# Attention in front of two expert layers: q in 1 KB runs, score groups over two row tiles, denominators from a tiny column

## The chip, the cores and the metric

The kernel runs on one core of a Trainium2 chip. The metric is the device time of one execution in microseconds (us). Of the kernel before there are three runs, 450.9, 451.15 and 452.35 us, with a median of 451.15 us. One execution was taken by the hardware profiler; its times are those of the rows below.

Names of the engines: PE is the matrix engine (TensorE), PEld its weight loads, DVE the vector engine, ACT the scalar engine, POOL is GpSimd, SP the engine that issues most DMAs. A row of the profile names the line of the kernel (L1475 is line 1475), the operation, and the tiles that are written and read.

## The reference, cut to what matters

```python
def _attn_ref(q, k, v):            # (8, 8, 576, 64): batch, head, token, dim
    k_p = k.reshape(B, H, 72, 8, D).mean(axis=3)
    v_p = v.reshape(B, H, 72, 8, D).mean(axis=3)
    scores = scale * np.matmul(q, k_p.transpose(0, 1, 3, 2))
    attn = np.exp(scores - np.max(scores, axis=-1, keepdims=True))
    attn = attn / (np.sum(attn, axis=-1, keepdims=True) + 1e-09)
    return np.matmul(attn, v_p)

def _moe_ref(x, phi, w1, w2):      # x: (4608, 512), 8 experts of 4 slots
    logits = x @ phi
    d = softmax(logits, axis=0);  c = softmax(logits, axis=1)
    slot_input = (d.T @ x).reshape(8, 4, 512)
    slot_out[e] = np.maximum(slot_input[e] @ w1[e], 0.0) @ w2[e]
    return c @ slot_out.reshape(32, 512)

def _moe2_ref(x, w_in, w_out, g_ln):
    h = x @ w_in
    solu = h * softmax(h)
    return (layer_norm(solu) * g_ln) @ w_out
```

Keys and values are averaged over 8 tokens, so a row of scores has 72 entries for each head. The first layer's dispatch softmax `d` runs over all tokens of all batches.

## The kernel before, in words

All data is float32. Three stages follow each other.

**Attention, batch by batch (to some 178 us).** A batch has 576 tokens in five row tiles. Tiles 0 to 3 have 128 rows, row p of tile t being token 4p + t; tile 4 holds the last 64 tokens, four heads on partitions 0 to 63 and four on 64 to 127. q comes in four DMAs of 256 KB a batch (runs of 64 numbers, 256 B) and two of 64 KB for tile 4; each of the five has a semaphore of its own. k and v come as two DMAs each, are folded in three levels (`fold`: levels 0 and 1 of width 1280 and 640, level 2 of 320) by POOL, a few of them by DVE, and are transposed by PE (`kT_t`, `vT_t`). ACT copies kT into `kblk`: for each of four pairs of heads a block diagonal of 128 rows and 2 x 72 columns, so one matmul gives the scores of two heads. The softmax tile `attn` has for each row tile four pairs of 147 columns: one column of ones, and for each head 72 scores and one column that holds 1e-9 (`TINY`).

For each tile the steps are these, and each engine runs them in an order written out by hand (`step(b, par, t)` on every engine, t from 1 to 5, where t = 5 is tile 0 of the next batch):

- PE `qT_t` (L1393): transposes q, four pairs of heads; ACT `qT_evac` copies the result to SBUF
- PE `scores` (L1412, tile 4: L1408); DVE `sub_max` takes the maximum (L1033) and subtracts it while writing into `attn` (L1039); ACT `exps` (L728); DVE `sums` takes the sum (L1046) and the reciprocal (L1051)
- POOL `norm` (L577) multiplies `attn` with the reciprocals and counts `attn_ready` up by one
- PE `aT_t` (L1475, tile 4: L1471) waits for `attn_ready` and transposes the 588 columns of the tile in blocks of 128; ACT `aT_evac` copies them
- PE `lt_t` (L1499) gives the logits with the v-weighted phi (`vphi`), ACT `lt_evac`, PE `l_t` (L1506), DVE `logit_evac` (L1058)

In step t, PE issues in this order: qT(t+3), scores(t+2), lt(t-1), aT(t), l(t-1), with `kT_t`, `vT_t`, `wphi_t`, `vphi_t`, `v72_t`, and the dispatch work of the batch before (`dat_t`, `datT_t`, `slot_t`, `lmax_t`, `mb_t`) between them. In step t, POOL issues norm(t+1), and behind it the folds: `v_fold` levels 1 and 2 in step 1, `k_fold` level 0 in step 3, levels 1 and 2 in step 4, `v_fold` level 0 in step 5. DVE begins step t with sums(t+1) and sub_max(t+2); in step 1 `vphi_evac` stands before them and `new_max` (L1083, L1087) behind them, in step 4 of the batches from 1 on `vT_copy` (L1065) stands at the end. ACT copies one half of kT in step 1 and one in step 2, before `lt_evac` and `exps` of the step.

`dat_t` multiplies the dispatch weights with `attn`, whose column of ones gives the denominator of the dispatch softmax.

SP issues the loads in one queue: at the start k(0), q tiles 0 and 1, v(0), q tiles 2 and 3, then, as POOL and DVE free the buffers, k(1), the rest of q(0), q tile 0 of batch 1, v(1), the rest of q(1), k(2). From batch 3 on it also loads expert weights into free places; ten halves of 2 MB fit before PE has used the first. The start has instructions of its own: at its end PE issues scores(2), vT_t, aT(0) of batch 0, and then step 1. There are a few transposes without use (`keep_clock`, L1560) in its gaps.

**Expert layer (to some 222 us).** PE multiplies the slots with w1 and w2 of each expert (`hid_t` L1698, `so_t` L1720). The load of weight half n (L446, L436, L438) waits until PE has used the half n - 10.

**Output layer (to the end).** 36 tiles of 128 tokens; the products of L1835 to L1837 keep PE full.

Of the kernel before, what the change touches and what calls it, by code (L numbers as in the profile page):

```python
# [29 lines left out]
F32 = mybir.dt.float32  # L30
F32R = mybir.dt.float32r
ALU = mybir.AluOpType
# [3 lines left out]
P = 128  # L36
B, H, S, D = 8, 8, 576, 64
POOL = 8
# [14 lines left out]
PAIR = 1 + 2 * HEAD  # L53
# [28 lines left out]
def build(nc, q, k, v, phi, w1, w2, w_in, w_out, g_ln, out):  # L82
    with ExitStack() as ctx:
# [36 lines left out]
        qb, ql = [bump("qb0", [P, 4, DM])], [bump("ql0", [P, DM])]  # L120
# [9 lines left out]
        qb.append(bump("qb1", [P, 4, DM]))  # L130
# [4 lines left out]
        kblk = [bump("kblk0", [P, PAIRS, 2 * SP])]  # L135
# [7 lines left out]
        kblk.append(bump("kblk1", [P, PAIRS, 2 * SP]))  # L143
# [9 lines left out]
        alpha = [bump(f"alpha{i}", [P, 1]) for i in range(2)]  # L153
        dlog = bump("dlog", [P, TILES, SLOTS])
# [29 lines left out]
        col_parts = bump("col_parts", [P, DM])  # L184
        m_hi = bump("m_hi", [P, FF // 4], F32R)
# [9 lines left out]
        csum = bump("csum", [P, B * TILES])  # L195
        csum1 = bump("csum1", [P, B * TILES])
        crec = bump("crec", [P, B * TILES])
# [5 lines left out]
        hid = [bump(f"hid{i}", [P, 2 * P]) for i in range(2)]  # L203
        hz = [bump(f"hz{i}", [P, FC, SLOTS]) for i in range(2)]
        pick = bump("pick", [P, 4, 5 * SLOTS], F32R)
        c_first = bump("c_first", [P, 2 * P])
# [37 lines left out]
        q_main = q[:, :, 0:4 * P, :].rearrange("b h (p t) d -> b t p h d", t=4)  # L244
# [72 lines left out]
        def head_sums(par, t):  # L317

            return pair_rows(par, t)[:, :, 1:].rearrange("p j (h c) -> p j h c", c=HEAD)

        def head_cols(par, t):
            return head_sums(par, t)[:, :, :, 0:SP]
# [25 lines left out]

        def kblk_half(par, hh):
            return kblk[par][hh * D:(hh + 1) * D, :, hh * SP:(hh + 1) * SP]  # L350
# [49 lines left out]
        def _(sp):  # L400
# [23 lines left out]
            def load_q(b, par, tiles=range(TILES)):  # L424
                for t in tiles:
                    if t < 4:
                        sp.dma_start(qb[par][:, t, :].rearrange("p (h d) -> p h d", h=H), row(q_main[:, t], b)).then_inc(sem(f"q_in{par}{t}"), 16)
                        continue
                    for hh in range(2):
                        sp.dma_start(ql[par][LEFT * hh:LEFT * (hh + 1), 0:DM // 2].rearrange("p (h d) -> p h d", d=D),  # L430
                                     row(q_left[:, :, H // 2 * hh:H // 2 * (hh + 1), :], b)).then_inc(sem(f"q_in{par}{t}"), 16)
# [36 lines left out]
            for b in range(1, 7):  # L468
# [4 lines left out]
                if b >= 3:  # L473
                    load_w((b - 3) // 2, (b - 3) % 2)
# [1425 lines left out]
```

## Time and profile before

| what | value |
|---|---|
| median of three runs | 451.15 us (450.9 to 452.35) |
| span of the profiled execution | 449.2 us |
| busy in the span: PE, PEld | 431.4 us (96%), 335.0 us (75%) |
| busy: DVE, ACT, POOL | 316.9 (71%), 267.4 (60%), 251.0 us (56%) |
| chain that ended last | PE 75%, DVE 7%, ACT 6%, DMA 6%, issue 3% |
| DMA | 91.71 MB in 125951 packets, 105176 of them under 512 B |
| granted TensorE clock, mean | 1.000 |

Busy time is the time in which an engine has an instruction under way. The shares are means over the three stages; the text on a stage reads that stage. In a timeline row the first number is the start in us from the span's start and the second the duration; x5 means that five instructions in a row are merged, and what stands in brackets is the idle time just before on that engine and who ended it.

### The profile page before, as it was taken

Reading aid. Unit: us, or ns where it says so; the run is one execution under the profiler, and the core shown is the slowest. Engines: PE = TensorE matmul, PEld = TensorE weight load, DVE = VectorE, ACT = ScalarE, POOL = GpSimd, SP = SyncE. Lnnn points to the kernel's source line nnn. Section 1 sums busy time; section 2 is a strip of 40 time slices with the busy share of each in tenths; the row PEclk is TensorE's granted clock in tenths of the full one; section 3 lists DMA queues with packets and bytes.
Section 4 is the critical chain, followed back from the end, with each engine's and each line's share of the span. In section 5 each row is a group of like instructions: output and inputs, shape, how many; then the busy total and the mean of one; then the engine's idle time right before and its main releaser. Section 6 shows DMA issues by size and latency. Waiting matters only on the chain.

```text
span 449.2 us, 10103 instructions
## 1 busy us (share of the span) xinstructions
PE 431.4 (96%) x3492; PEld 335.0 (75%) x3492; DVE 316.9 (71%) x558; ACT 267.4 (60%) x604; POOL 251.0 (56%) x347
## 2 busy tenths in 40 slices
PE   6899999999999998999899999999999999999997
PEld 6676787778778775445578788888888888888886
DVE  5888697877879665736598987777777777777311
ACT  2588878778787854134387665655565555666310
POOL 2569977878887230112034336766766667666540
PEclk9999999999999999999999999999999999999999
DMA  8969959898999998999500276676666766666642
GB/s 258 296 190 239 257 151 267 329 283 279 341 211 359 388 393 285 392 389 396 207 1 24 48 163 118 132 144 137 134 136 140 141 134 134 132 118 136 154 81 47
DMA packets 125951, 91.71 MB, mean 204 GB/s; under 512 B 105176, under 2 KB 105440, under 8 KB 124000
## 3 DMA queue, kind: packets, MB, share of 16 engines
q1 hardware_dynamic: 120752, 82.08, 66.8%
q10 hardware_dynamic: 5168, 9.24, 6.0%
q8 instruction: 17, 0.28, 0.3%
q14 instruction: 14, 0.11, 0.1%
HBM read 66.13 MB, written 9.44 MB: 168 GB/s over the span
## 4 chain that ended last, share of the span: by engine, by line
PE 75%; DVE 7%; ACT 6%; DMA 6%; issue 3%; POOL 1%; SPq 1%; DVEq 0%; ACTq 0%
PE banks L1835 13%; PE banks L1837 13%; PE banks L1836 13%; PE banks L1412 5%; DMA wslot<-in_moe_w 5%; PE banks L1475 3%; PE banks L1393 3%; PE banks L1807 3%; ACT vpad L685 2%; PE banks L1499 2%; PE banks L1535 2%; PE banks L1698 2%; PE banks L1506 2%; PE banks L1720 2%; DVE attn L1039 1%
## 5 line engine op out<-in xcount | busy, mean ns | idle before, releaser
L1835 PE MATMUL banks<-wo_hi,uh 128*128 128x512 f32 x280 | 109.6, 391 | 0.1
L1837 PE MATMUL banks<-wo_hi,ul 128*128 128x512 f32 x280 | 109.0, 389 | 0.0
L1836 PE MATMUL banks<-wo_lo,uh 128*128 128x512 f32 x280 | 108.9, 389 | 0.0
L653 POOL TENSOR_TENSOR ul<-u_col,uh 128x1024 fp32r<-128x1024 f32 x30 | 72.2, 2407 | 16.2 <-ACT uh L685 15.0
L577 POOL TENSOR_TENSOR attn<-attn,srec 128x576 f32<-128x576 f32 (+1 forms) x40 | 43.2, 1082 | 39.6 <-DVE srec L1051 39.4
L950 ACT ACTIVATE sq<-u,st 128x1024 f32<-128x1024 f32 x36 | 41.5, 1153 | 39.9 <-DVE u L1284 39.9
L1835 PEld LDWEIGHTS banks<-wo_hi,uh 128*128 128x128 f32 x280 | 52.6, 188 | 11.4 <-DVE ul L1301 0.5
L1837 PEld LDWEIGHTS banks<-wo_hi,ul 128*128 128x128 f32 x280 | 52.5, 188 | 11.0
L1836 PEld LDWEIGHTS banks<-wo_lo,uh 128*128 128x128 f32 x280 | 52.6, 188 | 10.7
L1284 DVE SCALAR_TENSOR_TENSOR u<-banks,ex 128x1024 f32<-128x1024 f32 x35 | 42.7, 1223 | 22.3 <-ACT ex L941 22.2
L1274 DVE TENSOR_REDUCE st<-banks 128x1 f32<-128x1024 f32 x35 | 42.6, 1218 | 17.5 <-PE banks L1807 17.5
L941 ACT ACTIVATE ex<-banks,st 128x1024 f32<-128x1024 f32 x35 | 39.0, 1114 | 17.1 <-DVE st L1274 16.7
L685 ACT ACTIVATE uh<-u_col 128x1024 fp32r<-128x1024 f32 x30 | 31.8, 1060 | 28.4 <-DMA u_col<-u_blk 14.5
L1315 DVE TENSOR_SCALAR osb<-banks,rs 128x512 f32<-128x512 f32 x35 | 26.0, 742 | 19.2 <-PE banks L1837 19.2
L1412 PE MATMUL banks<-kblk,qT 128*128 128x144 f32 x256 | 37.8, 291 | 1.0 <-DVE attn L1039 0.9
L1294 DVE STREAM_TRANSPOSE u_blk<-u 128x1024 f32<-128x1024 f32 x30 | 37.4, 1246 | 1.9
L1412 PEld LDWEIGHTS banks<-kblk,qT 128*128 128x128 f32 x256 | 33.1, 190 | 3.7 <-issue 3.5
L639 POOL TENSOR_SCALAR st<-st 128x1 f32<-128x1 f32 x36 | 6.9, 190 | 51.6 <-ACT sq L950 51.3
L1033 DVE TENSOR_REDUCE smax<-banks 128x8 f32<-128x576 f32 (+1 forms) x40 | 27.4, 685 | 10.9 <-PE banks L1412 10.5
L728 ACT ACTIVATE attn<-attn 128x576 f32<-128x576 f32 (+1 forms) x40 | 25.5, 636 | 14.8 <-DVE attn L1039 14.4
L1046 DVE TENSOR_REDUCE ssum<-attn 128x8 f32<-128x584 f32 (+1 forms) x40 | 27.8, 694 | 4.9 <-ACT attn L728 4.6
L685 ACT ACTIVATE aT<-banks 128x512 f32<-128x512 f32 (+1 forms) x80 | 28.7, 403 | 2.1 <-PE banks L1475 1.0
(197 smaller groups left out, 792.8 us busy)
## 6 DMA issues: line engine op xcount, KB each, us to landing
wslot<-in_moe_w SPq DMA_DIRECT2D x13, 2048.0 KB, 13.6
u_col<-u_blk SPq DMA_DIRECT2D x240, 64.0 KB, 2.2
qb<-in_q SPq DMA_DIRECT2D x32, 256.0 KB, 6.3
out<-osb ACTq DMA_DIRECT2D x32, 256.0 KB, 2.5
vraw<-in_v SPq DMA_DIRECT2D x8, 640.0 KB, 5.4
kraw<-in_k SPq DMA_DIRECT2D x7, 640.0 KB, 5.9
vraw<-in_v SPq DMA_DIRECT2D x8, 512.0 KB, 4.0
kraw<-in_k SPq DMA_DIRECT2D x7, 512.0 KB, 5.0
```

Source lines behind the costliest of these rows:

```text
L577: pool.tensor_tensor(a, a, per_head(srec[bit(tile)], t)[:, :, :, None].to_broadcast([P, tile_pairs(t), 2, SP]), ALU.mult) \
L653: pool.tensor_tensor(ul[par][:, :, :].rearrange("p c (q t) -> p (c q) t", q=4), v, uh[par][:, :, :].bitcast(F32).rearrange("p c (q t) -> p ...
L685: return act.activation(o, i, ACT.Copy, scale=scale)
L941: act.activation(ex[par][:, :, :], h_banks(par), ACT.Exp, bias=st[k % STATS]["nmax"][:, :], accum_out=st[k % STATS]["den"][:, :]).then_inc ...
L950: act.activation(sq[par][:, :], u[k % URING][:, :], ACT.Square, scale=-float(FF), bias=st[k % STATS]["usum"][:, :], accum_out=st[k % STATS ...
L1274: dve.tensor_reduce(st[k % STATS]["nmax"][:, :], h_banks(k % 2), AX.XY, ALU.max, negate=True).then_inc(sem("nmax"), 1)
L1284: dve.scalar_tensor_tensor(u[k % URING][:, :].rearrange("p (a n) -> p a n", a=2), h_banks(par), 1.0, ex[par][:, :, :], ALU.mult, ALU.mult, ...
L1294: dve.transpose(u_blk[slot][:, :, :, k % 2, :].rearrange("p c q t -> p (c q) t"), u[k % URING][:, :].rearrange("p (b f) -> p b f", f=BLK)) \
L1412: last = pe.matmul(s_view[:, j, 0:2 * SP], qT[bit(tile)][:, j, :], kblk[par][:, j, :], start=True, stop=True)
L1835: pe.matmul(ps[4 + par], uh[par][:, c, :], wo_hi[:, c, :], start=(c == 0), stop=False)
L1836: pe.matmul(ps[4 + par], uh[par][:, c, :], wo_lo[:, c, :], start=False, stop=False)
L1837: last = pe.matmul(ps[4 + par], ul[par][:, c, :], wo_hi[:, c, :], start=False, stop=(c == FC - 1))
```

## The change

1. q of a batch comes in one DMA of 1 MB: partition p gets for each head the tokens 4p to 4p + 3, a run of 256 numbers (1 KB). For batch 0 it is cut in two DMAs of 512 KB (runs of 512 B), token offsets 0 and 1 first; tile 0 now waits for 512 KB. SP issues all of q(1) ahead of v(1).
2. A group of scores ("unit") takes four heads of two token offsets instead of eight heads of one. Unit t of the first four has heads 4(t mod 2) to 4(t mod 2) + 3 of the offsets 2(t div 2) and the next. The transposed q has on its 128 rows one head at two offsets, so `kblk` holds for each head a block diagonal of that head twice: 8 blocks in place of 4. ACT's and DVE's copies of kT have twice the elements (64x256 where they had 64x128). The tile of 64 rows takes its pairs out of the same buffer with a stride of three.
3. The unit writes into `attn` its half of the columns of two row tiles. `sub_max`, `exps`, `sums` and `norm` work on `unit_cols` or `unit_sums`, four heads x two tiles x 72 (73) columns. `aT_t` of row tile 0 waits for the norms of units 0 and 1, that of tile 1 too; tiles 2 and 3 wait for units 2 and 3 (`units_of`).
4. The column of ones goes. The denominators are the sums over a TINY column, divided by TINY at the end. A pair has 146 columns, the row tile 584, its last block 72 (from 76).
5. Three small buffers of the later stages lie elsewhere (`hid`, `c_first`, `csum` and its kin).

The order of instructions on PE, DVE, ACT and POOL is as before.

```diff
-        q_main = q[:, :, 0:4 * P, :].rearrange("b h (p t) d -> b t p h d", t=4)
+        q_main = q[:, :, 0:4 * P, :].rearrange("b h (p t) d -> b p h (t d)", t=4)
...
+        def unit_sums(par, t):
+            if t == TILES - 1:
+                return pair_rows(par, t).rearrange("p j (h c) -> p j h c", c=HEAD)
+            first = GROUP_HEADS * HEAD * (t % 2)
+            return attn[:, par, t - t % 2:t - t % 2 + 2, first:first + GROUP_HEADS * HEAD].rearrange("p a (h c) -> p h a c", c=HEAD)
+        def unit_cols(par, t):
+            return unit_sums(par, t)[:, :, :, 0:SP]
+        def units_of(b, t):
+            return b * TILES + (TILES if t == TILES - 1 else t - t % 2 + 2)
...
         def kblk_half(par, hh):
-            return kblk[par][hh * D:(hh + 1) * D, :, hh * SP:(hh + 1) * SP]
+            return kblk[par][hh * D:(hh + 1) * D, :, hh, :]
+        def kblk_pair(par, j):
+            return kblk[par][:, 2 * j:2 * j + 2, :, :].rearrange("p h a c -> p (h a) c")[:, 0::3, :]
...
+            def load_q(b, par):
+                sp.dma_start(qb[par][:, :, :], row(q_main, b)).then_inc(sem(f"q_in{par}"), 16)
+            def load_first_q(n):
+                c = slice(2 * D * n, 2 * D * (n + 1))
+                sp.dma_start(qb[0][:, :, c], row(q_main, 0)[:, :, c]).then_inc(sem("q_in0" if n else "q_first"), 16)
...
             load_first_k()
-            load_q(0, 0, (0, 1))
+            load_first_q(0)
             load_v(0)
-            load_q(0, 0, (2, 3))
+            load_first_q(1)
...
-            load_q(0, 0, (4,))
-            load_q(1, 1, (0,))
+            load_left_q(0, 0)
             sp.dma_start(g8[:, :], g_v).then_inc(sem("g_in"), 16)
             sp.wait_ge(sem("v_pooled"), 1)
+            load_q(1, 1)
             load_v(1)
-            load_q(1, 1, (1, 2, 3, 4))
+            load_left_q(1, 1)
...
-                a = head_cols(tile[1], t)
+                a = unit_cols(tile[1], t)
                 pool.wait_ge(sem("srec"), num(tile) + 1)
...
-                dve.memset(pair_cols[:, :, :, 0], 1.0)
...
-                    i = ql[par][:, j * P:(j + 1) * P] if t == 4 else qb[par][:, t, j * P:(j + 1) * P]
+                    i = ql[par][:, j * P:(j + 1) * P] if t == 4 else qb[par][:, GROUP_HEADS * (t % 2) + j, P * (t // 2):P * (t // 2 + 1)]
...
-                        last = pe.matmul(s_view[:, j, 0:2 * SP], qT[bit(tile)][:, j, :], kblk[par][:, j, :], start=True, stop=True)
+                        last = pe.matmul(s_view[:, j, 0:2 * SP], qT[bit(tile)][:, j, :],
+                                         kblk[par][:, GROUP_HEADS * (t % 2) + j, :, :].rearrange("p a c -> p (a c)"), start=True, stop=True)
...
             def aT_t(tile):
-                pe.wait_ge(sem("attn_ready"), num(tile) + 1)
+                pe.wait_ge(sem("attn_ready"), units_of(b, t))
```

## Rows read from the trace of the kernel before

**Rows 1.** The page's first part: busy us, share of the span, instructions.

```profile
PE 431.4 (96%) x3492; PEld 335.0 (75%) x3492; DVE 316.9 (71%) x558; ACT 267.4 (60%) x604; POOL 251.0 (56%) x347
```

**Rows 2.** The chain of work that ended last: start, duration, what.

```profile
195.80 20.35 DMA wslot<-in_moe_w
```

**Rows 3.** Timeline of SP: the first weight load that waits for PE's products.

```profile
179.31 1.77 SPq L446 DMA_DIRECT2D wslot<-in_moe_w  x4
```

**Rows 4.** Windows: busy by engine, then PEclk, DMA share, GB/s.

```profile
75.00:150.00 75.00, 73.53 (x909) 58.02 (x910) 60.97 (x140) 59.29 (x183) 57.05 (x41) 1.00 0.97 304
90.00:95.00 5.00, 4.87 (x63) 3.54 (x61) 2.98 (x7) 3.75 (x12) 4.11 (x4) 1.00 1.25 231
140.00:145.00 5.00, 5.00 (x60) 3.69 (x60) 4.83 (x12) 3.71 (x12) 4.74 (x5) 1.00 1.03 409
175.00:180.00 5.00, 4.71 (x83) 3.04 (x75) 3.31 (x11) 2.14 (x5) 0.00 (x0) 1.00 0.68 188
```

**Rows 5.** Timeline: scores of tile 1, its norm, and the transposes of tile 0.

```profile
72.07 1.25 PE L1412 MATMUL banks<-kblk,qT 128*128 128x144 f32 x8
...
77.10 1.15 POOL L577 TENSOR_TENSOR attn<-attn,srec 128x576 f32<-128x576 f32 x1 [1.60 <-DVE srec L1051]
...
77.44 0.77 PE L1475 MATMUL banks<-ident,attn 128*128 128x128 f32 x5
```

**Rows 6.** Timeline: the norm of tile 3 and the transposes of tile 2.

```profile
83.39 1.06 DVE L1087 TENSOR_TENSOR slot_max<-lmax_new,slot_max 128x1 f32<-128x1 f32 x1
...
85.56 0.76 PE L1475 MATMUL banks<-ident,attn 128*128 128x128 f32 x5
...
85.63 1.15 POOL L577 TENSOR_TENSOR attn<-attn,srec 128x576 f32<-128x576 f32 x1 [0.24 <-DVE srec L1051]
```

**Rows 7.** Timeline of batch 7: norms of tiles 1 and 3, transposes of 0 and 2.

```profile
155.55 1.15 POOL L577 TENSOR_TENSOR attn<-attn,srec 128x576 f32<-128x576 f32 x1 [3.68 <-DVE srec L1051]
...
156.24 0.76 PE L1475 MATMUL banks<-ident,attn 128*128 128x128 f32 x5
...
163.10 1.15 POOL L577 TENSOR_TENSOR attn<-attn,srec 128x576 f32<-128x576 f32 x1 [2.02 <-DVE srec L1051]
...
163.58 0.77 PE L1475 MATMUL banks<-ident,attn 128*128 128x128 f32 x5
```

**Rows 8.** Timeline of batches 0 and 1: transposes (PE) and POOL's work.

```profile
17.91 0.71 PE L1475 MATMUL banks<-ident,attn 128*128 128x128 f32 x5
...
20.07 2.29 POOL L577 TENSOR_TENSOR attn<-attn,srec 128x576 f32<-128x576 f32 x1 [3.81 <-DVE srec L1051]
...
22.50 0.74 PE L1475 MATMUL banks<-ident,attn 128*128 128x128 f32 x5
...
26.04 2.92 POOL L386 TENSOR_TENSOR vraw<-vraw 128x1280 f32<-128x1280 f32 x1
...
26.77 0.77 PE L1475 MATMUL banks<-ident,attn 128*128 128x128 f32 x5
...
28.91 1.16 POOL L577 TENSOR_TENSOR attn<-attn,srec 128x576 f32<-128x576 f32 x1
...
32.35 1.22 PE L1412 MATMUL banks<-kblk,qT 128*128 128x144 f32 x8 [0.50 <-DVE attn L1039]
...
38.16 0.77 PE L1475 MATMUL banks<-ident,attn 128*128 128x128 f32 x5
...
40.30 1.15 POOL L577 TENSOR_TENSOR attn<-attn,srec 128x576 f32<-128x576 f32 x1
```

**Rows 9.** Groups of ACT by form, 40 to 157 us: busy, mean ns, idle before.

```profile
L685 ACT ACTIVATE kblk<-banks 64x128 f32<-64x128 f32 x24 | 6.5, 271 | 8.1 <-PE banks L1419 7.8
...
L685 ACT ACTIVATE datT<-banks 72x256 f32<-72x256 f32 x6 | 2.3, 375 | 0.0
```

**Rows 10.** Line L1560's weight loads (ns min/median/max), from 2 and from 11 us.

```profile
L1560 PEld LDWEIGHTS banks<-ident x26: 140/230/230, 2.0 to 6.6; 128*128 128x128 f32 x26
...
L1560 PEld LDWEIGHTS banks<-ident x12: 139/140/142, 11.1 to 12.3; 128*128 128x128 f32 x12
```

More of the change, by code:

```diff
@@ L52 @@
 HEAD = SP + 1
-PAIR = 1 + 2 * HEAD
+PAIR = 2 * HEAD
+GROUP_HEADS = H // 2
 LEAD = 6
@@ L134, in build @@
         attn_end = place[0]
-        kblk = [bump("kblk0", [P, PAIRS, 2 * SP])]
+        kblk = [bump("kblk0", [P, H, 2, SP])]
         vpad = bump("vpad", [P, PAIRS, PAIR])
@@ L153, in build @@
         alpha = [bump(f"alpha{i}", [P, 1]) for i in range(2)]
+        dlog_at = place[0]
         dlog = bump("dlog", [P, TILES, SLOTS])
@@ L184, in build @@
         col_parts = bump("col_parts", [P, DM])
+        hid = [at(f"hid{i}", [P, 2 * P], F32, place[0] + i * size([P, 2 * P])) for i in range(2)]
         m_hi = bump("m_hi", [P, FF // 4], F32R)
@@ L194, in build @@
         cmax = bump("cmax", [P, B * TILES])
-        csum = bump("csum", [P, B * TILES])
-        csum1 = bump("csum1", [P, B * TILES])
-        crec = bump("crec", [P, B * TILES])
+        csum, csum1, crec = (at(n, [P, B * TILES], F32, dlog_at + i * size([P, B * TILES])) for i, n in enumerate(("csum", "csum1", "crec")))
+        c_first = at("c_first", [P, 2 * P], F32, place[0])
         mean_ff = bump("mean_ff", [P, P])
@@ L422, in load_v, with load_left_q @@
                 load_rows(vraw, v_rows, b, sem("v_in"))
[L424 to L431, printed above, removed]
+            def load_q(b, par):
[3 more added lines that the diff above has]
+                sp.dma_start(qb[0][:, :, c], row(q_main, 0)[:, :, c]).then_inc(sem("q_in0" if n else "q_first"), 16)
+            def load_left_q(b, par):
+                for hh in range(2):
+                    sp.dma_start(ql[par][LEFT * hh:LEFT * (hh + 1), 0:DM // 2].rearrange("p (h d) -> p h d", d=D),
+                                 row(q_left[:, :, H // 2 * hh:H // 2 * (hh + 1), :], b)).then_inc(sem(f"ql_in{par}"), 16)
             def load_w(e, layer):
@@ L725, in exps @@
             def exps(tile):
-                a = head_cols(tile[1], tile[2])
+                a = unit_cols(tile[1], tile[2])
                 act.wait_ge(sem("s_sub"), num(tile) + 1)
@@ L994, in _ @@
             dve.memset(kraw[:, ODD, :], 0.0).then_inc(sem("raw_zero"), 1)
-            dve.memset(kblk[0][:, :, :], 0.0)
+            dve.memset(kblk[0][:, :, :, :], 0.0)
             for hh in range(2):
@@ L1407, in scores @@
                             r = slice(LEFT * hh, LEFT * (hh + 1))
-                            last = pe.matmul(s_view[r, j, 0:2 * SP], qT[bit(tile)][:, j, r], kblk[par][:, LPAIRS * hh + j, :],
+                            last = pe.matmul(s_view[r, j, 0:2 * SP].rearrange("p (a c) -> p a c", c=SP), qT[bit(tile)][:, j, r], kblk_pair(par, LPAIRS * hh + j),
                                              start=True, stop=True, tile_position=(0, LEFT * hh))
```

67 lines of the change are left out of this document (36 added, 31 removed).

## Prediction, written before the changed kernel was run

> **What bounds the kernel now.** I read the busy table first [rows 1]: TensorE (PE) is busy 96% of the span, the other engines are not near that. The 5 us windows split the span: until about 178 us the attention runs, to 216 us the expert weights stream, and the last 230 us are the output matmuls of L1835 to L1837, which the change doesn't touch. In the middle stage the chain has one piece of DMA of 20.35 us that starts at 195.8 [rows 2]. It doesn't reach back into the attention: between 175 and 180 us the transfers fell to 188 GB/s [rows 4], because SP was waiting for PE to free weight buffers. The last 14.7 MB (six loads of 2 MB for experts 5 to 7, and w_in) are issued from 179.3 us on, when PE has read the first part of the first weights [rows 3], and until 216.2, in 36.9 us, they move at 398 GB/s. So a microsecond that PE loses before 178 us is a microsecond of the total, and a microsecond that DMA gains there is not, unless PE was waiting for it. In the attention stage the waits of PE name DVE, ACT and "issue", and a DMA only for the very first q.
>
> So I ask of each edit: does PE, in its written order, get to an instruction whose input is now later?
>
> **The wait that changes.** aT_t transposes one row tile of the softmax. Before, tile t needed norm(t) alone. After, a group of scores fills half of the columns of two row tiles, so tiles 0 and 2 need norm(t) and norm(t+1); tiles 1, 3 and 4 need what they needed. No order of instructions is changed. norm(t+1) is issued on POOL in the same step as aT(t), and the rows show them abreast.
>
> *Tile 0 in the steady loop* [rows 5]. scores(1) start on PE at 72.07 and end at 73.32; maximum, exp, sum and reciprocal follow, and the norm runs from 77.10 to 78.25. aT(0) starts at 77.44. With 0.1 us from POOL's end to PE's start (22.36 and 22.50 in [rows 8]) it would wait to 78.35: 0.91 us. Everything in this chain hangs on scores(1), which PE issues before, so it moves along with PE and the wait comes back in every batch. Batches 2 to 6 show 0.86, 0.91, 0.89, 0.91 and 0.90: 4.5 us.
>
> *Tile 2* [rows 6]. norm(3) runs from 85.63 to 86.78, aT(2) starts at 85.56: 1.32 us. The five batches give 1.23 or 1.32, 6.3 us together. What is queued behind the waiting aT(t) on PE is all of it: l_t, v72 or vphi, the next qT and scores. PE idles only 1.5 us in the 75 us from 75 to 150 [rows 4], so nothing gives the time back. Nothing covers the stall either, since PE is the bound.
>
> *Batch 7* has no folds beside it [rows 7]: 156.70 + 0.1 - 156.24 = 0.56, and 164.25 + 0.1 - 163.58 = 0.77. Sum 1.3 us.
>
> *Start, batch 0* [rows 8]. aT(0) ran at 17.91; norm(1) ends at 22.36, so it would wait 4.55 us. Before, aT(1) followed at 22.50 with the waits for ACT's copies (vpad, wphi) between them. The same steps follow after, and I take 0.85 of the waits as absorbed: +3.7 (bounds 3.0 and 4.55). Then aT(2), at 26.77, needs norm(3), which stands on POOL behind norm(2) and v_fold(1,0) (26.04, 2.92 us) and ends at 30.07: +3.4. POOL's whole queue starts from norm(2), which is itself late by 3.7, so this adds in full: +7.1.
>
> *Batch 1*: norm(1) ends at 41.45 behind two folds, aT(0) was at 38.16: 3.39, of which 0.5 comes back, since PE idled that long before the scores at 32.35: +2.9. For aT(2) POOL has had time to catch up by then and the loop's 1.1 is left. +4.0 (bounds 2 and 6.5).
>
> **The other parts.** (1) k's blocks: each head twice, so the copies of kT have 256 elements where they had 128. ACT's 64x128 took 271 ns, a 72x256 375 ns [rows 9]; four such and two small ones make +0.24 in each of the two steps in which they run. In step 1 the copy of lt stands behind them and PE's l_t behind that; in step 2 the wait of aT(2) covers it. For six batches 0 to 1.4 us, taken as 1.0. (2) First q: 512 KB must land where 256 KB had. At 231 to 409 GB/s [rows 4] the extra is 0.6 to 1.1 us; a part of it is hidden by k's chain, which scores(0) also needs; the first kblk copies are longer by 0.25. Start +0.7 (0 to 1.3). (3) v(1) is issued behind 1 MB of q. POOL reached it at 26.04 [rows 8] and will come at about 29.7; v(1) is issued some 17.5 us in, and q and v, 2.2 MB, even at 231 GB/s have landed 9.6 us later. Nothing; without that cover it would be 1 us. SP's later order is the same, and q is needed 15 us after it is issued. (4) q in runs of 1 KB: fewer packets. In the stretch with q, 231 GB/s kept DMA full, while weights ran at 409 [rows 4]. So 1.05 MB falls from 4.5 to 2.6 us, some 1.9 us a batch, off the path. (5) Column of ones gone: 146 for 147 columns, a last block of 72 for 76, the memsets a little different, all hidden by the first loads; 0, at most 0.2 either way. (6) Element counts of DVE, ACT and POOL are unchanged, only the stride between runs of 72 is larger; no row shows this form. Bound below nothing: excluded, since the lengths are the same; above: POOL's own slowest norm, 2.29 us for 1.15 (beside a DVE fold) [rows 8]. I take 0, as 31 of 32 norms of this size need 1.15 to 1.16 with strides of 73 already. That row is a rival below.
>
> **The clock.** After the change PE has a hole of 4.3 us at 18 us and two of 3 in the next 15. The granted clock of the page is 1.0 throughout, its upper level, but in the first 5 us a weight load of 128 columns took 230 ns and at 11 us 140 ns [rows 10], so PE is slower after rest. If the holes do this, the 3 to 5 us of PE work on the path around them take up to twice as long: 0 to 5 us. I take 1.5.
> The Trainium skill (TensorE: Matmul & The Clock Gate, Part 1) says the same of PE at rest: it falls from 2.4 to 1.2 GHz and needs activity to come back; by it the 5 rather than the 0 would hold.
>
> **Sum.** 7.1 + 4.0 + 4.5 + 6.3 + 1.3 + 1.0 + 0.7 + 1.5 = 26.4 us. I take 0.5 off for idle time that PE has in the last batch and gives back. The profiled run has a span of 449.2 us, 1.95 under the median of 451.15: 449.2 + 25.9 + 1.95 = 477 us, 5.7% slower.
>
> **Rivals.**
> *The loop pays nothing.* norm(3) is late because DVE's slot_max (1.06 us for one column [rows 6], beside a fold on POOL) stands before the sum, and the vT copy before that of tile 1. If the folds no longer collide with these, or the producers run ahead while PE waits, the loop's 11 us mostly go: 477 - 11 - 1 = 465. For: POOL and DVE gain slack. Against: both chains hang on scores that PE issues, and the collisions are in the chains themselves.
> *DMA was the bound* (the other side). If the stream to 216 us was backed up all through, as the full window at 140 suggests [rows 4], four batches of q beside weights would give back 4 x 1.9 = 7.6 us: 443.5. It decides if PE's waits for norms are hidden, for then nothing is against it. Against: the gap at 175 to 180, and no wait of PE for a load.
> The Trainium skill (DMA: Bandwidth & Descriptors, Why small descriptors are slow) speaks for this saving: 27% overhead at 256 B, 9% at 1 KB by its count of beats. An estimate from the page would be 0.4 us a batch, less than the row.
> *The norms get slower*: POOL's new stride costs as the 2.29 did, 1.1 more in each of 14 waits: 477 + 15 = 492. Half of that, 485, is as likely.
> *The clock stays low* through the first 40 us: 5 to 8 us in place of 1.5, 482 to 485.
> *The change doesn't do what it says*: the runs of q might still move slowly; this changes nothing above, as q is off the path.
>
> **Chances.** Stalls as summed (467 to 482): 0.66. Loop pays nothing or half (455 to 467): 0.13. Clock stays low (482 to 486): 0.09. Norms slower (over 486): 0.06. DMA, faster: 0.05; 0.01 for no change. The likeliest alone spans 467 to 482; the range takes in part of the second and the third: 463 to 486. A measurement tells 0.3%, 1.4 us, from no change. Faster 0.05, same 0.01, slower 0.94.
>
> **What would show it.** In the profile after: POOL's norm named as what PE waits for at the transposes of tiles 0 and 2, some 0.9 and 1.3 us each, twice a batch and not three times; the longest in the first 45 us; hid_t(0) beginning at some 204 in place of 178.6; the DMA piece of 20 us still there. A mean norm over 1.3 us shows the third rival, weight loads of 230 ns after 22 us the fourth. Wrong from the root: transposes of tiles 0 and 2 that start without a wait.

## Result, and the profile after

The changed kernel takes 481.1 us (median of four runs, 478.3 to 482.7) where the kernel before takes 451.0 in the same comparison: a ratio of 1.064, with a 95% interval of 1.060 to 1.067. The profiled execution has a span of 479.2 us against 449.2, so 30.0 us more. The forecast was 477 us, in a range of 463 to 486.

Lines of the page after, which answer to [rows 1]: the busy table, the granted clock in 40 slices of 12 us each, the shares of the chain that ended last, and the groups of the transposes `aT_t` (L1504 now) and of the norm (L602 now).

```profile
PE 439.4 (92%) x3492; PEld 341.6 (71%) x3492; DVE 316.4 (66%) x556; ACT 272.2 (57%) x604; POOL 251.6 (53%) x347
...
PEclk9977799999999999899999999999999999999999
...
PE 58%; POOL 15%; issue 10%; DVE 8%; DMA 5%; ACT 2%; SPq 0%; POOLq 0%; DVEq 0%
...
L602 POOL TENSOR_TENSOR attn<-attn,srec 128x576 f32<-128x576 f32 (+1 forms) x40 | 43.4, 1085 | 68.2 <-DVE srec L1077 68.2
...
L1504 PE MATMUL banks<-ident,attn 128*128 128x128 f32 (+1 forms) x160 | 26.3, 299 | 23.3 <-POOL attn L602 23.3
```

Three things stand in them. PE idled 23.3 us before its transposes, and POOL's norm ended that; in the kernel before there is no such wait. POOL, 1% of the chain before, has 15% of it. And PE's busy time itself grew by 8.0 us with the same 3492 instructions, while the granted clock shows slices of 0.7 in the first 60 us and one of 0.8 at 192 us: the other part of the loss is not a wait.

The timeline of the transposes answers to [rows 5 to 8] (start, duration, in brackets the idle time before; in batches 0 and 1 tiles 0, 1 and 2, in batch 2 tiles 0 and 2), and behind it the first matmul of the experts.

```profile
23.08 1.30 PE L1504 MATMUL banks<-ident,attn 128*128 128x128 f32 x5 [4.51 <-POOL attn L602]
29.30 0.77 PE L1504 MATMUL banks<-ident,attn 128*128 128x128 f32 x5
37.07 1.30 PE L1504 MATMUL banks<-ident,attn 128*128 128x128 f32 x5 [3.39 <-POOL attn L602]
...
53.24 1.30 PE L1504 MATMUL banks<-ident,attn 128*128 128x128 f32 x5 [3.23 <-POOL attn L602]
...
64.34 0.74 PE L1504 MATMUL banks<-ident,attn 128*128 128x128 f32 x5 [0.75 <-POOL attn L602]
...
77.19 0.74 PE L1504 MATMUL banks<-ident,attn 128*128 128x128 f32 x5 [0.91 <-POOL attn L602]
...
85.65 0.74 PE L1504 MATMUL banks<-ident,attn 128*128 128x128 f32 x5 [1.03 <-POOL attn L602]
...
208.21 1.93 PE L1727 MATMUL banks<-wslot,slotT 128*32 128x256 f32 x32
```

In the kernel before, tile 0 of batch 2 and the first matmul of the experts:

```profile
58.04 0.77 PE L1475 MATMUL banks<-ident,attn 128*128 128x128 f32 x5
...
178.61 1.93 PE L1698 MATMUL banks<-wslot,slotT 128*32 128x256 f32 x32
```

The waits sit at tiles 0 and 2 and nowhere else. After the three long ones the five transposes take 1.30 us in place of 0.74: they ran at a lower clock. Against before, the transposes of batch 0, tile 0 are 5.2 us later, those of batch 2, tile 0 19.2 (77.19 and 58.04) and the first expert matmul 29.6 (208.21 and 178.61). From there to the end only 0.4 us are added: the loss is all in the attention. The weight stream's last piece is still there and about as long as in [rows 2], 19.59 us for 20.35:

```profile
226.46 19.59 DMA wslot<-in_moe_w
```

Windows of 5 us of the kernel after that lie under the full clock (busy by engine, then granted clock, DMA share, GB/s); in the kernel before no window of the attention lies under it.

```profile
20.00:25.00 5.00, 1.92 (x9) 1.92 (x10) 1.89 (x3) 0.95 (x4) 4.28 (x3) 0.72 1.06 397
25.00:30.00 5.00, 5.00 (x29) 3.56 (x27) 1.34 (x4) 2.98 (x9) 0.37 (x1) 0.59 0.80 220
...
35.00:40.00 5.00, 2.93 (x15) 2.84 (x16) 0.92 (x2) 1.09 (x3) 1.92 (x2) 0.59 0.00 2
40.00:45.00 5.00, 5.00 (x38) 4.47 (x37) 2.54 (x6) 2.67 (x7) 0.08 (x1) 0.73 0.00 2
...
50.00:55.00 5.00, 1.77 (x11) 1.76 (x10) 1.70 (x4) 1.54 (x6) 4.92 (x4) 0.80 0.89 276
55.00:60.00 5.00, 5.00 (x31) 3.45 (x33) 3.49 (x9) 1.89 (x6) 3.09 (x3) 0.52 0.35 147
...
190.00:195.00 5.00, 4.04 (x36) 2.93 (x37) 2.34 (x8) 1.99 (x7) 1.70 (x2) 0.79 0.13 39
195.00:200.00 5.00, 4.91 (x81) 3.67 (x79) 0.70 (x4) 2.91 (x11) 0.76 (x4) 0.87 0.57 213
```

Each of the first three pairs lies on and behind one of the three long waits. The fourth lies in the last batch, behind waits of 0.54, 0.56 and 0.76 us that follow each other within 3.5 us. Between 25 and 30 us PE is busy for the whole window with 29 matmuls; a full window at full clock has 60 [rows 4].

Two groups by form, ACT's copies of kT (from 40 us on), and POOL's norm in the same stretch:

```profile
L710 ACT ACTIVATE kblk<-banks 64x256 f32<-64x256 f32 x24 | 9.1, 378 | 10.4 <-PE banks L1448 10.1
...
L602 POOL TENSOR_TENSOR attn<-attn,srec 128x576 f32<-128x576 f32 x28 | 32.3, 1154 | 34.2 <-DVE srec L1077 34.2
```

The copies are 0.107 us longer than in [rows 9], as estimated from the 72x256 there. The norm takes 1154 ns for 1150 before: the new stride costs POOL nothing.

### The profile page after: what moved, and what is told of

It is laid out like the page before. It is cut to its first block, busy times and chain, and to the rows that moved or that the text cites. A ratio compares the mean times of both kernels' runs of the same rounds, so it can differ in the third digit from the quotient of the medians.

```text
span 479.2 us, 10078 instructions
## 1 busy us (share of the span) xinstructions
PE 439.4 (92%) x3492; PEld 341.6 (71%) x3492; DVE 316.4 (66%) x556; ACT 272.2 (57%) x604; POOL 251.6 (53%) x347
## 3 DMA queue, kind: packets, MB, share of 16 engines
q1 hardware_dynamic: 96832, 82.08, 58.8%
## 4 chain that ended last, share of the span: by engine, by line
PE 58%; POOL 15%; issue 10%; DVE 8%; DMA 5%; ACT 2%; SPq 0%; POOLq 0%; DVEq 0%
PE banks L1864 13%; PE banks L1865 13%; PE banks L1866 13%; POOL attn L602 5%; DMA wslot<-in_moe_w 4%; POOL kraw L406 3%; POOL vraw L406 3%; PE banks L1836 3%; PE banks L1440 3%; PE banks L1504 2%; PE banks L1727 2%; PE banks L1749 2%; POOL kraw L409 2%; DVE ssum L1072 2%; PE banks L1564 1%
## 5 line engine op out<-in xcount | busy, mean ns | idle before, releaser
L602 POOL TENSOR_TENSOR attn<-attn,srec 128x576 f32<-128x576 f32 (+1 forms) x40 | 43.4, 1085 | 68.2 <-DVE srec L1077 68.2
L1504 PE MATMUL banks<-ident,attn 128*128 128x128 f32 (+1 forms) x160 | 26.3, 299 | 23.3 <-POOL attn L602 23.3
L1440 PE MATMUL banks<-kblk,qT 128*128 128x144 f32 x256 | 40.7, 306 | 0.8 <-DVE attn L1065 0.4
L1341 DVE TENSOR_SCALAR osb<-banks,rs 128x512 f32<-128x512 f32 x35 | 26.0, 742 | 19.2 <-PE banks L1866 19.2
L1440 PEld LDWEIGHTS banks<-kblk,qT 128*128 128x128 f32 x256 | 35.9, 203 | 3.4 <-issue 3.0
L1504 PEld LDWEIGHTS banks<-ident,attn 128*128 128x128 f32 (+1 forms) x160 | 17.6, 144 | 28.5 <-issue 28.4
```

The source lines that it names most:

```text
L602: pool.tensor_tensor(a, a, per_head(srec[bit(tile)], t)[:, :, :, None].to_broadcast([P, tile_pairs(t), 2, SP]), ALU.mult) \
L1440: last = pe.matmul(s_view[:, j, 0:2 * SP], qT[bit(tile)][:, j, :], kblk[par][:, GROUP_HEADS * (t % 2) + j, :, :].rearrange("p a c -> p (a ...
L1504: last = pe.transpose(b_aT[k // 4][0:m, (k % 4) * P:(k % 4 + 1) * P], attn[:, par, t, k * P:k * P + m], ident[:, :])
```

## Experiments

"Before" is measured anew beside each group of runs (451.4 to 452.9 us). No experiment leaves out a part of the computation; those that add transposes without use change nothing of it.

### Is it the wait alone?

The kernel before in everything, q, blocks and column of ones too; only the condition of `aT_t` is that of the change:

```diff
-                pe.wait_ge(sem("attn_ready"), num(tile) + 1)
+                pe.wait_ge(sem("attn_ready"), b * TILES + (TILES if t == TILES - 1 else t - t % 2 + 2))
```

> The kernel before with one line changed: the transposes of row tiles 0 and 2 wait until the norms of tiles 0 and 1, or 2 and 3, are done, as in the changed kernel. Loads, layout, k's blocks and the column of ones stay as before. Theory 1 (the wait is the loss): 478 to 482 us, the same as the changed kernel, with PE's clock falling in the first 60 us. Theory 2 (the longer copies of kT, the strides over two tiles and the order of loads have a share): 470 to 477, and the rest must be found in those parts. Theory 3 (the waits only show where something else is late): under 458.

Measured: 482.1 us (478.9 to 484.1), ratio 1.067 (1.062 to 1.072). Two of PE's waits in its trace, the first number being the total in us, then the count and the longest:

```profile
PE banks L1475 <- POOL attn L577: 23.5, 16, 4.3
PE banks L1499 <- DVE c_all L1058: 1.1, 2, 0.7
```

The changed kernel has 23.3 us in 16 waits for the norm. So the wait for the second norm is enough to make the whole loss, and the sum of all other parts, those of DMA included, can't be told from nothing in the medians. That doesn't mean that each of them is nothing: the second row is a wait that the kernel before has too and the changed kernel has not, and in this trace the clock falls behind it in batches 3 and 5, which it doesn't in the changed kernel's. The sections below come back to it.

### Do q's longer runs buy anything?

The changed kernel, but each load of q cut again into pieces with runs of 64 numbers (256 B), as many bytes and as many packets as before (the two loads of the first q are cut in the same way):

```diff
-                sp.dma_start(qb[par][:, :, :], row(q_main, b)).then_inc(sem(f"q_in{par}"), 16)
+                for t in range(4):
+                    c = slice(D * t, D * (t + 1))
+                    sp.dma_start(qb[par][:, :, c], row(q_main, b)[:, :, c]).then_inc(sem(f"q_in{par}"), 16)
```

> The changed kernel with q loaded in four DMAs of 256 KB a batch again, runs of 256 B, into the new layout; nothing else. Theory 1 (q is off the path): 480 to 482.5 us, as the changed kernel, though the queue time of the packets rises again from 59% to some 67%. Theory 2 (runs of 1 KB gave time back that the waits hide): slower than the changed kernel, 484 to 489, by 1.9 us for each of up to four batches that have weights beside them.

Measured: 481.8 us (480.4 to 482.0), the same as the changed kernel. The queue that carries the loads, in the kernel after and then in this one:

```profile
q1 hardware_dynamic: 96832, 82.08, 58.8%
```

```profile
q1 hardware_dynamic: 120752, 82.08, 63.0%
```

The longer runs save 24,000 packets and 4.2 points of the sixteen engines' span, or some 20 us with all sixteen busy, 2.5 us a batch; nothing of it reaches the end. The prediction had 1.9 from rows of the trace before. The Trainium skill (DMA: Bandwidth & Descriptors, Why small descriptors are slow) is right that small runs cost DMA time, but the estimate of 0.4 us a batch from its count is too low; here DMA had that time to spare. Longer runs in a kernel without the new wait were not tried; what speaks against a gain there is that the kernel before has no wait of PE for a load between the first q and the expert weights.

### How much of the start is clock?

The changed kernel with transposes without use ahead of the three long waits, so that PE works while it would idle. It still can't pass before the norm is there.

```diff
+            keep_clock(b_tail, 34)
             aT_t((0, 0, 0))
...
+                    if first and t in (2, 5):
+                        keep_clock(b_tail, 26)
                     aT_t(tile)
```

> The changed kernel with useless transposes in three places where PE waits for POOL: 34 ahead of the transposes of tile 0 of batch 0, 26 ahead of tile 2 of batch 0, 26 ahead of tile 0 of batch 1. The waits themselves stay. Theory 1 (some 5 us of the loss are PE's clock, which falls in the holes of 4.5, 3.4 and 3.2 us): 474 to 477 us, granted clock about 1.0 in every window to 60 us, and the transposes after the holes at 0.75 in place of 1.30 us for five. Theory 2 (the clock falls, but PE is waiting for others at that time anyway): 479 to 481, with the clock up. Theory 3 (more was lost by the transposes than they save): over 482.

Measured: 474.7 us (473.6 to 476.6), ratio 1.052 (1.050 to 1.055), 6.4 us less than the 481.1 of the changed kernel. Timeline of its transposes (batch 0, tiles 0, 1, 2; batch 1, tile 0) and the first expert matmul:

```profile
23.09 0.74 PE L1504 MATMUL banks<-ident,attn 128*128 128x128 f32 x5 [0.81 <-POOL attn L602]
26.88 0.77 PE L1504 MATMUL banks<-ident,attn 128*128 128x128 f32 x5
34.68 0.74 PE L1504 MATMUL banks<-ident,attn 128*128 128x128 f32 x5 [0.38 <-POOL attn L602]
...
48.41 0.74 PE L1504 MATMUL banks<-ident,attn 128*128 128x128 f32 x5 [0.39 <-POOL attn L602]
...
199.61 1.93 PE L1730 MATMUL banks<-wslot,slotT 128*32 128x256 f32 x32
```

The first transposes start when they did (23.09 and 23.08), the wait is as long; but tile 1 follows after 3.8 us in place of 6.2, and no window of this trace is under the full clock. (This is the fastest of the four executions; the others had a mean clock of 0.991 to 0.996.) Each of the three long waits had cost another 2.4 to 2.7 us after it was over: against this trace the changed kernel is 2.4 us late at tile 1 of batch 0 (29.30 and 26.88), 5.1 at tile 3 (42.99 and 37.91) and 7.8 at tile 1 of batch 1 (60.42 and 52.67). This trace at full clock is also the one in which the other terms of the sum can be read.

The same transposes in the kernel that has only the new wait (first experiment), to see whether the two agree when the clock is steadier:

> The kernel before with the wait alone for all batches, and the useless transposes in the same three holes of the start. Set beside the changed kernel with these transposes (474.7 us) it leaves only the loads, the layout and the longer kT copies as a difference, without the noise of the clock. Theory 1 (these parts are worth nothing): 473.5 to 476. Theory 2 (they cost the 1.7 us that the forecast had for the first q and the kT copies): 472 to 473.3.

```diff
+            keep_clock(b_tail, 34)
             aT_t((0, 0, 0))
...
-                pe.wait_ge(sem("attn_ready"), num(tile) + 1)
+                pe.wait_ge(sem("attn_ready"), b * TILES + (TILES if t == TILES - 1 else t - t % 2 + 2))
```

Measured: 474.9 us (474.6 to 479.5), ratio 1.050 (1.047 to 1.053), against 474.7 and 1.052. They agree, but the clock was not steady in all executions: the one of 479.5 us is the one in the trace, and there it fell at tile 2 of batches 1, 3 and 5.

### Does the loop pay what the waits show?

The kernel before, with the wait for both norms only from tile 2 of batch 1 on; the start is as before:

```diff
-                pe.wait_ge(sem("attn_ready"), num(tile) + 1)
+                both = t in (0, 2) and not (isinstance(b, int) and (b == 0 or (b == 1 and t == 0)))
+                pe.wait_ge(sem("attn_ready"), num(tile) + (2 if both else 1))
```

> The kernel before with the wait for both norms only from tile 2 of batch 1 on; the start keeps its old waits, and with them the holes of 3 to 4.5 us are gone. Theory 1 (the loop's part is the sum of its waits, 0.9 + 1.14 a batch, less the 0.33 a batch for which PE waited before anyway): 451.4 + 5 x 1.73 + 1.3 + 3 for tile 2 of batch 1, some 464 us. Theory 2 (nothing comes back): 466 to 467. Theory 3 (the holes of 1.2 us are enough to let the clock fall in some batches, as two transposes of 1.14 and 1.30 us in the run with the wait alone hint): 466 to 470, with a granted clock under 1.0 somewhere from 60 us on and runs that differ by more than 2 us.

Measured: 471.7 us (470.0 to 474.3), ratio 1.045 (1.040 to 1.049). With the wait at tile 2 alone:

```diff
+                both = t == 2 and not (isinstance(b, int) and b == 0)
```

> As the run before this one, but only tile 2 waits for both norms (from batch 1 on), tile 0 never. Theory 1 (each wait adds by itself): the five waits of 1.14, less 0.33 each, 0.77 in batch 7 and 3 in batch 1: some 8 us, 459 to 460. Theory 2 (when tile 0 doesn't wait, POOL and DVE are less ahead and tile 2 waits longer, or the other way round): 457 or 462.

Measured: 465.8 us (464.3 to 467.8), ratio 1.031 (1.028 to 1.035). Both are 6 to 8 us more than the waits' sums of 464 and 459 to 460, and more than any theory on record allowed them (470 and 462); 1.5 us of it is that the kernel before took 452.9 beside these runs and not 451.4. Windows of the first of the two:

```profile
90.00:95.00 5.00, 3.04 (x33) 2.33 (x31) 4.09 (x10) 3.42 (x10) 4.15 (x4) 0.94 0.21 52
95.00:100.00 5.00, 5.00 (x50) 4.54 (x49) 1.64 (x5) 2.78 (x8) 2.83 (x2) 0.71 1.00 308
```

and its transposes of batch 3 (tile 0, tile 2) and batch 4 (tile 0), with the wait for `c_all` that comes just ahead of tile 2:

```profile
85.41 0.74 PE L1476 MATMUL banks<-ident,attn 128*128 128x128 f32 x5 [0.87 <-POOL attn L577]
...
92.39 0.60 PE L1500 MATMUL banks<-aT,vphi 128*32 128x128 f32 x10 [0.67 <-DVE c_all L1058]
...
94.61 1.30 PE L1476 MATMUL banks<-ident,attn 128*128 128x128 f32 x5 [1.29 <-POOL attn L577]
...
109.01 0.74 PE L1476 MATMUL banks<-ident,attn 128*128 128x128 f32 x5 [0.88 <-POOL attn L577]
```

Behind idle times of 0.67 and 1.29 us, 0.9 us apart, the transposes took 1.30 us again, the clock was down. The wait at tile 2 of batch 1 (3.12 us) lowers it too (0.66 from 50 to 55 us). The same pair of waits stands in batches 3 and 5 of every kernel with the old layout: of the eight pairs in the four such traces whose loop was not filled the clock fell behind six. In no trace did it fall in batches 2 to 6 behind a wait for the norm that had no such neighbour, and 18 of those were of 1.20 to 1.26 us.

### Filling the loop's waits

First with too many transposes, 12 before tile 0 and 16 before tile 2 of every later batch and 12 in the wait for the first q, in the kernel with the busy start:

```diff
+                    elif t in (2, 5):
+                        keep_clock(b_aT[0], 16 if t == 2 else 12)
                     aT_t(tile)
```

> The changed kernel with transposes without use in every hole that it has: the wait for the first q (12), the three waits of the first 45 us (34, 26, 26, as in the run with busy holes), and in every later batch before the transposes of tile 0 (12) and of tile 2 (16). The waits for the norms stay. Theory 1 (the loop's cost is the wait itself, and the clock was lost in the first holes only): the time of the run with busy holes again, 474 to 475 us, with the same scatter of some 3 us. Theory 2 (short holes in the loop let the clock fall in some executions): 471 to 473, the median near the lowest time of the run with busy holes, all runs within 1 us, granted clock 1.00 in every window. Theory 3 (the added transposes stand in PE's way because they run longer than the wait): slower than 475.

Measured: 481.2 us (479.4 to 482.2). And the same in the kernel with the loop's wait alone:

```diff
+                    if t in (2, 5) and not first:
+                        keep_clock(b_aT[0], 16 if t == 2 else 12)
```

> The kernel before, with the wait for both norms from tile 2 of batch 1 on, plus transposes without use: 12 in the wait for the first q, 12 before the transposes of tile 0 and 16 before those of tile 2. Without them this kernel took 471.7 us where the waits summed to 464. Theory 1 (the rest is granted clock lost in holes of 1 to 3 us): 464 to 466 us and a clock of 1.00 in every window. Theory 2 (the rest is a wait that the sum did not hold, a ripple to other engines): 470 to 472, unchanged. Between the two, 467 to 469, each would be a part.

Measured: 472.4 us (471.9 to 474.0). These two did not tell the theories apart, since the filling was longer than the wait. In the first of them, tile 0 of batch 3:

```profile
92.18 1.53 PE L1589 MATMUL banks<-ident 128*128 128x128 f32 x12
93.54 0.71 PE L1504 MATMUL banks<-ident,attn 128*128 128x128 f32 x5
```

12 transposes take 1.36 us from the first to the real ones behind them, 0.113 each, and the real ones follow without any wait: I had counted 0.055. The batch grew from 21.4 to 22.4 us. With 7 and 9 of them, none for the first q:

```diff
-                        keep_clock(b_aT[0], 16 if t == 2 else 12)
+                        keep_clock(b_aT[0], 9 if t == 2 else 7)
```

> As the run with transposes in all holes, but as many as fit into the wait: one of them took 0.11 us back to back there (12 in 1.37 us, 16 in 1.8), so 7 before the transposes of tile 0 (0.8 us in a wait of 0.9 to 1.0) and 9 before those of tile 2 (1.0 in 0.9 to 1.25); none for the first q; 34, 26, 26 at the start as before. The loop should return from 22.35 us a batch to 21.4. Theory 1 (the last 6 us of the run before this one were only transposes that ran longer than the waits, and the loop's holes cost nothing beside themselves): 474 to 476, as with the start's holes filled alone. Theory 2 (the loop's holes cost clock): 471 to 473.

Measured: 475.2 us (473.1 to 478.8), ratio 1.054 (1.050 to 1.058), the same as with the start's waits filled alone.

> The kernel before with the wait for both norms from tile 2 of batch 1 on, and 7 and 9 transposes in the loop's waits, none elsewhere. Its unfilled twin took 471.7 us at a mean clock of 0.982 to 0.989, where the waits summed to 464, and the one with 12 and 16 had 0.993 to 0.996 and a batch of 22.2 us where 21.4 would be without overlong fillers: some 5 to 6 us of its 472.4. Theory 1 (the rest is clock): 466 to 468 and a mean clock of 0.995 or more. Theory 2 (the rest is a ripple to other engines): 470 to 472.

Measured: 467.7 us (466.3 to 468.9), ratio 1.035 (1.032 to 1.038), 4.0 us less than its unfilled twin, with the same condition on the norms. The three transposes that stood above (batch 3 tiles 0 and 2, batch 4 tile 0), and its window there:

```profile
84.11 0.74 PE L1476 MATMUL banks<-ident,attn 128*128 128x128 f32 x5
...
93.31 0.74 PE L1476 MATMUL banks<-ident,attn 128*128 128x128 f32 x5 [0.15 <-POOL attn L577]
...
106.13 0.74 PE L1476 MATMUL banks<-ident,attn 128*128 128x128 f32 x5
```

```profile
95.00:100.00 5.00, 5.00 (x74) 3.99 (x73) 2.77 (x6) 3.72 (x10) 3.87 (x3) 1.00 1.16 282
```

From tile 0 to tile 0 it is 22.02 us here and 23.60 there: one fall of the clock costs 1.6 us. The waits for `c_all` (0.67 and 0.4 us) are the same in both. So the excess over the waits' sum in the two kernels above is in good part clock. In the kernel with the busy start, filling gained nothing that can be measured; its trace without the filling has no window under full clock either, so there was little to gain. Its executions still scatter (473.1 to 478.8 us). The trace is of one of 475.0 and has windows of 0.73 at 10 us, behind the wait for the first q, and of 0.68 in the last batch, where no transposes were put; that the scatter comes from these was not shown.

### Can the order of the instructions hide the wait?

The changed kernel with the transposes later on PE: at tile 2 `v72_t` and `l_t` go first, at tile 0 of the next batch `vphi_t` and `l_t`, from batch 1 on.

```diff
+                if late and t == 2:
+                    v72_t(b)
+                if late and t == 5:
+                    vphi_t(b + 1)
                 l_t(before)
+                if late:
+                    aT_t(tile)
```

> The changed kernel with another order on PE in the loop: the transposes of tile 2 are issued behind l_t of the tile before and v72_t, those of tile 0 of the next batch behind vphi_t and l_t. The start of batch 0 stays. Each of these gives 0.9 us of work into a wait of 0.9 to 1.25. Theory 1 (the waits cost because PE stands still, not because the chain is longer): the loop loses 0.1 to 0.5 in place of 1.7 us a batch, so 8 to 11 us less: 470 to 474 us. Theory 2 (the chain from scores to norm to transposes is itself the period, so what PE does in the hole doesn't matter): 479 to 482.

Measured: 472.0 us (470.6 to 473.3), ratio 1.046 (1.043 to 1.048). Its waits:

```profile
PE banks L1504 <- POOL attn L602: 9.3, 3, 4.5
PE banks L1488 <- ACT kblk L710: 3.2, 6, 0.5
PE banks L1477 <- ACT wphi L710: 3.0, 7, 0.7
```

The waits for the norms are gone from the loop; the three left are those of the start, the last now 1.4 us. But half of what they were comes back as waits of the instructions that moved ahead, for ACT's copies `kblk` and `wphi`: 6.2 us for 12.2 (23.3 less the three waits of the start). The batch takes 20.7 us, where the changed kernel has 21.4 and the kernel before 19.6.

With the start reordered too, on PE, ACT, POOL and DVE (the first two tiles' transposes both after norm(1), v's first folds behind the norms, the fold of k one step later):

```diff
+                    aT_t(before)
+                    keep_clock(b_tail, 3)
                     aT_t(tile)
...
-                if t == 4 and k_next:
+                if t == (5 if first else 4) and k_next:
```

> The changed kernel with the late transposes of the loop and with the start reordered as well: in batch 0 the transposes of tile 0 stand behind vphi_t and those of tile 2 behind v72_t and l_t, POOL does norm(3) ahead of v_fold(1,0) and norm(1) of batch 1 ahead of the last two k folds, DVE takes the scores ahead of its two v folds, ACT's order follows PE's. Theory 1 (all of the loss was PE standing before norms that its order didn't leave time for, and the clock that fell with it): 453 to 458 us, granted clock 1.0, no wait for POOL over 0.5 us. Theory 2 (the unit layout itself costs something in the start, where POOL is the bound): 460 to 466, with POOL still named in the first 60 us.

Measured: 467.9 us (465.5 to 469.4), ratio 1.033 (1.029 to 1.036). The waits for POOL are down to 1.5 us, and this is the fastest form with the new layout that was found; it doesn't reach the kernel before, nor the 460 to 466 that the more cautious theory had. Its first matmul waited 2.5 us for q, and its clock was at 0.50 between 10 and 15 us:

```profile
PE banks L1494 <- ACT kblk L711: 5.3, 7, 2.0
PE banks L1483 <- ACT wphi L711: 3.0, 7, 0.7
PE banks L1427 <- DMA qb<-in_q: 2.5, 1, 2.5
PE banks L1534 <- ACT aT L711: 1.9, 4, 0.7
PE banks L1510 <- POOL attn L602: 1.5, 2, 1.4
```

## Why the prediction was right, and which of its terms were off

The mechanism was the one that was forecast: tiles 0 and 2 wait for the norm of the tile behind, PE is the bound, and little gives the time back. The wait alone makes 482.1 us in the kernel before, and the changed kernel has 481.1. But that 477 lies within 1% is partly luck, because terms erred to opposite sides: the clock was some 7 us too small and the loop some 3 too large. The terms, read in the trace at full clock (span 471.8, so 22.6 us over before; the sum without the clock was 24.4):

- *Batch 0, +7.1 with +0.7 for the first q.* The transposes of tile 0 were to start at 17.91 + 0.7 + 4.55 = 23.16 and start at 23.09. Tile 1 was to be 4.4 late and is 4.4 late (26.88 and 22.50); tile 2 7.8 and is 7.9 (34.68 and 26.77). So the absorbed 0.85, POOL's queue behind the late norm and the first q hold to 0.1 us.
- *Batch 1, +4.0.* At its tile 0 the sum has 10.7, the trace 10.3 (48.41 and 38.16); at tile 0 of batch 2, with that tile's own 0.9, the sum has 12.7, the trace 11.9 (69.89 and 58.04). Too much by 0.8.
- *The loop, 10.8, and copies of kT, +1.0.* From tile 0 of batch 2 to tile 0 of batch 7 the sum has 10.4 for the waits (tile 2 five times, tile 0 five times, the last with 0.56) and up to 1.0 for the copies; the shift grows by 8.4 (11.9 to 20.3). The waits in the trace are 9.7: tile 0 as forecast, tile 2 at 1.02 and 1.25 in turn, not 1.23 and 1.32. Another 1.1 comes back right behind the waits: tile 1 follows tile 0 after 4.26 us in place of 4.55, tile 3 follows tile 2 after 3.73 in place of 3.82. The first experiment shows the same: a batch of it with waits of 2.08 us takes 21.27 where the kernel before takes 19.42, so 0.23 of the 2.08 is not paid. And 1.1 is a wait that the kernel before has at `lt_t` in batches 3 and 5 for DVE's `c_all`, and that is gone. I had taken PE's idle time in the loop, 1.5 us in 75, as too small to look through; most of it was this:

```profile
PE banks L1499 <- DVE c_all L1058: 1.1, 2, 0.7
```

It is not gone because DVE gains on PE while PE waits for norms, as the rival had it: in the first experiment PE waits as long, and the row is the same. It goes with an idle time of DVE ahead of `vphi_evac`, which has no releaser in the profile ("issue"): 0.49 us in batch 3 and 0.22 in batch 5 before and in the kernels with the wait added to it, none in the changed kernel. Batch 3 before, and in the changed kernel:

```profile
79.97 0.19 DVE L1070 COPY vphi<-banks 128x32 f32<-128x32 f32 x1 [0.49 <-issue]
```

```profile
100.23 0.19 DVE L1096 COPY vphi<-banks 128x32 f32<-128x32 f32 x1
```

Which part of the change takes it away, no run shows. The waits less these two amounts make some 7.4 us; the other 1.0 of the measured 8.4 is as large as the copies' term, and behind tile 1, where that term was expected, PE is in fact later (`l_t` starts 0.76 us after the transposes do, 0.60 in the first experiment). No run took the copies apart. So the rival that the loop pays nothing has little for it: of the 10.4 us of waits 9.7 were there, and 1.1 of these came back.
- *Batch 7, +1.3.* The waits are 0.54 and 0.76. Right. The first expert matmul is then 21.0 late (199.61 and 178.61), the end of this trace 22.6. The last 1.6 were in no term: PE waits 1.56 us for the last half of the expert weights, where it was 1.01 before, and once for POOL in the output layer, which neither the trace before nor that of the changed kernel has. In the changed kernel these stages add 0.4.

```profile
293.88 0.47 PE L1867 MATMUL banks<-wo_hi,uh 128*128 128x512 f32 x1 [0.82 <-POOL ul L678]
```

- *The clock, +1.5 (0 to 5).* It is the term that was mis-sized. At the first expert matmul the changed kernel is 8.6 us behind the trace at full clock (208.21 and 199.61): 7.8 from the three long waits, of which 0.5 comes back at tile 2 of batch 1 (a wait of 0.75 in place of 1.19), and 1.3 in the last batch, whose short waits were not looked at. At the end it is 7.4 (479.2 - 471.8), because the trace at full clock has the 1.6 above; 6.4 lie between the medians. The step that failed is the bound of "3 to 5 us of PE work around the holes". The clock is not low in the wait only, but for some microseconds of full work behind it (0.59 from 25 to 30 us, 0.52 from 55 to 60), and there the work takes up to twice as long. What was slow behind each hole cost 2.4 to 2.7 us, so behind the three 7.8 and not at most 5. The Trainium skill (TensorE: Matmul & The Clock Gate, Part 1) had the better direction: PE has to be busy again before the clock comes back. The rival "clock stays low" named 5 to 8 us as its condition; that condition is what came true, and only the loop's shortfall kept the time at 481, under its 482 to 485.
- *Norms slower.* 1154 ns for 1150: not so. *DMA was the bound.* The runs of 256 B put back give 481.8 for 481.1: not so, by an experiment and not only by argument. *The change doesn't do what it says.* It does; the packets fell from 120,752 to 96,832 in that queue.
- The place of the loss was right: the first expert matmul was to start at some 204 and starts at 208.2, the piece of 20 us stays (19.59), and the 204 lacks the clock's 7 and has the loop's 3 too much.

Open: of the two kernels that have the wait in the loop alone, the better filled one is at 467.7, where the waits sum to 464. Its trace has windows of 0.80 to 0.86 from 175 to 195 us, behind waits in the last batch, where nothing was filled. That this is all of the rest was not tried. Nor is it shown what DVE's idle time ahead of `vphi_evac` is, or why the clock fell behind six of the eight pairs of waits and not behind the other two.

## What to carry to other kernels

A layout that joins two tiles in one producer makes the consumer of the first wait for the second. Where the engine behind is the bound and both hang on what it issues itself, that wait comes back in every round, and it can be read off the timeline before the change: end of the second producer minus start of the first consumer. Price a hole on PE at its length and, if it is long or has another close beside it, at the slow work behind it as well; put work, useful or not, into the hole, but never more than the hole is long. And ask, before cheaper transfers are bought with a new wait, whether anything was waiting for the transfers.

## What the runs showed of the hardware

- The waits of 3.2 to 4.5 us let the granted clock fall and cost 2.4 to 2.7 us each beyond their length.
- Short idle times can do it too when they stand close together. In batches 2 to 6 the clock fell behind six of eight pairs of waits (0.40 to 0.67 us and, 0.9 us later, 1.29), and one such fall cost 1.6 us, more than the longer wait itself. It fell behind none of 18 waits of 1.20 to 1.26 us that stood alone; in batch 1 it fell once behind a lone wait of 1.29 (0.76 from 60 to 65 us, in the kernel before with the wait and the busy start). In the last batch of the changed kernel waits of 0.54, 0.56 and 0.76 us within 3.5 us were followed by windows of 0.79 and 0.87. The Trainium skill (TensorE: Matmul & The Clock Gate, HAM oscillation) warns of idle gaps that are longer than any wait in this loop; the rows here put the trouble lower.
- Transposes whose result nobody reads can hold the granted clock: with them in the three waits it read 1.00 in every window of the trace, and useless transposes that add work saved 6.4 us. Twelve in a row took 1.36 us, 0.113 each.
- The second norm took 2.29 us on POOL beside a fold of k on DVE (at 20.07 us before, at 20.65 after the change), where others take 1.15; the Trainium skill (SBUF — State Buffer, SBUF: two separate sides) describes an exclusive port pair of the two, which fits, but no run here took the fold away.
